# Token tiles of 512 columns in five groups and 448 in the sixth, and a last product by halves of its tokens

## What the kernel computes

```python
qn = q / (norm(q, axis=1) + 1e-06); kn = k / (norm(k, axis=1) + 1e-06)
a  = softmax(kn^T @ qn / tau)            # 256 x 256
x  = (v @ a)                             # 6016 x 256
x  = square(relu(x @ w_in1)) @ w_out1    # d_ff = 2048
y  = leaky_relu(x2 @ w_in2, 0.01) @ w_out2
```

## Time and profile before

| | us |
|---|---|
| median of 3 runs | 1021.57 |
| lowest and highest | 1021.54, 1021.75 |
| the profiled execution | 1021.69 |
| its span, first to last instruction | 1019.9 |
| TensorE busy | 1015.7 |
| VectorE busy | 724.0 |
| ScalarE busy | 673.3 |

### The profile page before, as it was taken

The page is one execution under the profiler, slowest core; times in us unless marked ns, Lnnn a source line. Parts: engine busy times, 40 slices in busy tenths (PEclk is TensorE's granted clock), DMA queues, the critical chain, the costliest instruction groups (busy, mean ns, idle before and its releaser), DMA issues.

```text
span 1019.9 us, 13177 instructions
## 1 busy us (share of the span) xinstructions
PE 1015.7 (100%) x4602; PEld 859.3 (84%) x4602; DVE 724.0 (71%) x1195; ACT 673.3 (66%) x1186; POOL 27.7 (3%) x35
## 2 busy tenths in 40 slices
PE   9999999999999999999999999999999999999998
PEld 8888888888888888888888888888888888888887
DVE  6999766667667666666558777867777777777665
ACT  6898877777777777777665556555555556555454
POOL 3700000000000000000000000000000000000000
PEclk9999999999999999999999999999999999999999
DMA  9800121130130131125361001002002002000001
GB/s 364 315 21 22 32 82 45 54 137 32 67 137 31 68 119 51 68 77 188 116 210 64 1 26 56 1 1 80 1 1 80 1 1 82 1 1 35 6 0 42
DMA packets 33874, 69.27 MB, mean 68 GB/s; under 512 B 2832, under 2 KB 18704, under 8 KB 33808
## 3 DMA queue, kind: packets, MB, share of 16 engines
q1 hardware_dynamic: 33232, 67.25, 18.9%
q10 hardware_dynamic: 576, 1.18, 0.3%
HBM read 44.56 MB, written 23.86 MB: 67 GB/s over the span
## 4 chain that ended last, share of the span: by engine, by line
PE 99%; DMA 0%; ACT 0%; ACTq 0%; issue 0%
PE psum L525 32%; PE psum L526 32%; PE psum L527 32%; PE psum L532 3%; DMA qk<-in_k 0%; ACT out_buf L1004 0%; PE psum L588 0%; PE psum L577 0%; ACTq L728 0%; PE psum L579 0%
## 5 line engine op out<-in xcount | busy, mean ns | idle before, releaser
L867 ACT ACTIVATE g_hi<-g 128x496 fp32r<-128x496 f32 (+1 forms) x384 | 237.3, 618 | 200.8 <-DVE g L1178 76.6
L1168 DVE TENSOR_TENSOR g_lo<-g,g_hi 128x496 fp32r<-128x496 f32 (+1 forms) x384 | 259.9, 677 | 137.5 <-ACT g_hi L867 135.3
L527 PE MATMUL psum<-g_hi,wout_lo 128*128 128x496 f32 (+1 forms) x768 | 295.4, 385 | 0.0
L526 PE MATMUL psum<-g_lo,wout_hi 128*128 128x496 f32 (+1 forms) x768 | 295.4, 385 | 0.0
L525 PE MATMUL psum<-g_hi,wout_hi 128*128 128x496 f32 (+1 forms) x768 | 295.4, 385 | 0.0
L526 PE MATMUL psum<-xop_lo,win_hi 128*128 128x496 f32 (+1 forms) x672 | 258.5, 385 | 0.0
L527 PE MATMUL psum<-xop_hi,win_lo 128*128 128x496 f32 (+1 forms) x672 | 258.5, 385 | 0.0
L525 PE MATMUL psum<-xop_hi,win_hi 128*128 128x496 f32 (+1 forms) x672 | 258.4, 385 | 0.0
L525 PEld LDWEIGHTS psum<-g_hi,wout_hi 128*128 128x128 f32 x768 | 144.2, 188 | 26.6
L527 PEld LDWEIGHTS psum<-g_hi,wout_lo 128*128 128x128 f32 x768 | 144.2, 188 | 26.5
L526 PEld LDWEIGHTS psum<-g_lo,wout_hi 128*128 128x128 f32 x768 | 144.2, 188 | 26.4
(11 more groups left out here) (104 smaller groups left out, 685.8 us busy)
## 6 DMA issues: line engine op xcount, KB each, us to landing
up_parts<-park_up SPq DMA_DIRECT2D x8, 896.0 KB, 4.2
qk<-in_q SPq DMA_DIRECT2D x15, 384.0 KB, 9.7
qk<-in_k SPq DMA_DIRECT2D x13, 384.0 KB, 11.1
stage_o<-in_w_out SPq DMA_DIRECT2D x16, 256.0 KB, 3.4
down_parts<-park_down SPq DMA_DIRECT2D x8, 512.0 KB, 2.8
raw<-in_vT SPq DMA_DIRECT2D x8, 496.0 KB, 4.9
x_tiles<-out_buf SPq DMA_DIRECT2D x8, 496.0 KB, 2.9
raw<-x_tiles SPq DMA_DIRECT2D x8, 496.0 KB, 4.1
```

The lines of the kernel that those rows point to most:

```text
L526: pe.matmul(out, a_hi, b_lo, start=False, stop=False, **more)
L527: last = pe.matmul(out, a_lo, b_hi, start=False, stop=stop and i == len(operands) - 1, **more)
L867: act.activation(g_hi[:, tile, 0:W], g[:, tile, 0:W], ACT.Copy).then_inc(g_hi_made[tile], 1)
L1168: dve.tensor_tensor(g_lo[:, tile, 0:W], g[:, tile, 0:W], g_hi[:, tile, 0:W].bitcast(F32), ALU.subtract).then_inc(g_split[tile], 1)
```

## The change

The widths become five groups of 512 columns and a last one of 448; they add up to the same 3008. Groups 1 to 4 and 7 to 10 get wider, groups 5 and 11 narrower. In the end `down_last` takes the place of `down` for C12: it does o = 0 whole (3 matmuls of 448 columns) and o = 1 in two halves of 224 columns, the second into another PSUM bank (`end_bank`, bank 3), into which ScalarE has first copied what is summed so far. VectorE copies o = 0 of the second tile instead of ScalarE. The halves are copied and stored each by itself, the first by SyncE's queue, the second by ScalarE's.

```diff
-    WIDTHS = [512, 496, 496, 496, 496, 512]
+    WIDTHS = [512, 512, 512, 512, 512, 448]
+    END = width(ALL_GROUPS - 1)
+    def end_tokens(h):
+        return bass.ds(2 * sum(WIDTHS[0:GROUPS - 1]) + END + h * END // 2, END // 2)
+        end_bank = banks[3][:, 0:END // 2]
+        end_seeded = sem("end_seeded")
+        end_done = [sem(f"end_done{h}") for h in range(2)]
 # SyncE, at the end
             for j in range(2):
                 sp.wait_ge(out0_made[j], ALL_GROUPS)
-                sp.dma_start(yT_b[:, 0, tokens(ALL_GROUPS - 1, j)], out_buf[:, 0, j, 0:width(ALL_GROUPS - 1)]
-                             ).then_inc(stored[j], 16)
+                sp.dma_start(yT_b[:, 0, tokens(ALL_GROUPS - 1, j)], out_buf[:, 0, j, 0:END]).then_inc(stored[j], 16)
+                sp.wait_ge(out1_made[j], ALL_GROUPS)
                 if j == 0:
-                    sp.wait_ge(out1_made[j], ALL_GROUPS)
-                    sp.dma_start(yT_b[:, 1, tokens(ALL_GROUPS - 1, j)], out_buf[:, 1, j, 0:width(ALL_GROUPS - 1)]
-                                 ).then_inc(stored[j], 16)
-            for j in range(2):
-                sp.wait_ge(stored[j], 16 * (ALL_GROUPS + 1))
+                    sp.dma_start(yT_b[:, 1, tokens(ALL_GROUPS - 1, j)], out_buf[:, 1, j, 0:END]).then_inc(stored[j], 16)
+                else:
+                    sp.dma_start(yT_b[:, 1, end_tokens(0)], out_buf[:, 1, j, 0:END // 2]).then_inc(stored[j], 16)
+            sp.wait_ge(stored[0], 16 * (ALL_GROUPS + 1))
+            sp.wait_ge(stored[1], 16 * (ALL_GROUPS + 2))
 # TensorE
+            def down_last():
+                m = 2 * (QUADS - 1) + ROW[C12]
+                pe.wait_ge(g_split[C12], WINDOWS)
+                three_passes(acc[0][1][:, 0:END], [(wout_hi[:, m, 0:P], wout_lo[:, m, 0:P], g_hi[:, C12, 0:END],
+                                                    g_lo[:, C12, 0:END])], start=False).then_inc(end_first, 1)
+                pe.wait_ge(end_seeded, 1)
+                for h, place in enumerate((acc[1][1][:, 0:END // 2], end_bank)):
+                    cols = slice(h * END // 2, (h + 1) * END // 2)
+                    three_passes(place, [(wout_hi[:, m, P:C], wout_lo[:, m, P:C], g_hi[:, C12, cols],
+                                          g_lo[:, C12, cols])], start=False, skip_group_check=True
+                                 ).then_inc(end_done[h], 1)
-            for tile in (C11, C22, C21, C12):
+            for tile in (C11, C22, C21):
                 down(WINDOWS - 1, tile)
+            down_last()
 # ScalarE, at the end (out_end and its three calls and the store are taken out)
+            act.wait_ge(down_done[C22], WINDOWS)
+            act.activation(end_bank, acc[1][1][:, END // 2:END], ACT.Copy).then_inc(end_seeded, 1)
+            act.wait_ge(end_first, 1)
+            act.wait_ge(stored[0], 16 * (ALL_GROUPS - 1))
+            act.activation(out_buf[:, 0, 0, 0:END], acc[0][0][:, 0:END], ACT.Copy).then_inc(out0_made[0], 1)
+            act.wait_ge(end_done[0], 1)
+            act.wait_ge(stored[1], 16 * (ALL_GROUPS - 1))
+            act.activation(out_buf[:, 1, 1, 0:END // 2], acc[1][1][:, 0:END // 2], ACT.Copy).then_inc(out1_made[1], 1)
+            act.wait_ge(end_done[1], 1)
+            act.activation(out_buf[:, 1, 1, END // 2:END], end_bank, ACT.Copy).then_inc(out1_made[1], 1)
+            act.wait_ge(out1_made[1], ALL_GROUPS + 1)
+            act.dma_start(yT_b[:, 1, end_tokens(1)], out_buf[:, 1, 1, END // 2:END]).then_inc(stored[1], 16)
 # VectorE, at the end, behind out_second(ALL_GROUPS - 1, 0)
+            dve.wait_ge(end_first, 2)
+            dve.wait_ge(stored[1], 16 * (ALL_GROUPS - 1))
+            dve.tensor_copy(out_buf[:, 0, 1, 0:END], acc[0][1][:, 0:END]).then_inc(out0_made[1], 1)
```

More of the change, by code:

```diff
@@ L638, in down @@
                     cut = slice(o * P, (o + 1) * P)
+                    read_early = Q == WINDOWS - 1 and tile == C22 and o == 1
                     last = three_passes(acc[o][j][:, 0:W], [(wout_hi[:, m, cut], wout_lo[:, m, cut],
@@ L641, in down @@
                                         start=quad == 0 and tile in (C11, C22),
-                                        stop=quad == QUADS - 1 and tile in (C21, C12))
-                    if Q == WINDOWS - 1 and o == 0 and tile in (C21, C12):
+                                        stop=quad == QUADS - 1 and tile in (C21, C12) or read_early)
+                    if Q == WINDOWS - 1 and o == 0 and tile == C21:
                         last.then_inc(end_first, 1)
                 last.then_inc(down_done[tile], 1)
+            def down_last():
[9 more added lines that the diff above has]
+                                 ).then_inc(end_done[h], 1)
             def wait_weights(Q, split):
@@ L995, in _ @@
             g_high(WINDOWS - 1, C12)
[L997 to L1004, removed]
-            out_end(0, 0, out0_made[0])
-            out_end(0, 1, out0_made[1])
-            out_end(1, 1, out1_made[1])
-            act.wait_ge(out1_made[1], ALL_GROUPS)
-            act.dma_start(yT_b[:, 1, tokens(ALL_GROUPS - 1, 1)], out_buf[:, 1, 1, 0:width(ALL_GROUPS - 1)]
-                          ).then_inc(stored[1], 16)
+            act.wait_ge(down_done[C22], WINDOWS)
[10 more added lines that the diff above has]
+            act.dma_start(yT_b[:, 1, end_tokens(1)], out_buf[:, 1, 1, END // 2:END]).then_inc(stored[1], 16)
         @block.vector
```

## The result

The changed kernel takes 1023.65 us (median of 18 runs, 1023.45 to 1024.08) against 1021.67 us for the kernel before (18 runs beside it). The ratio is 1.0018 with a 95% interval of 1.0012 to 1.0025: 2.0 us slower, outside the range that was forecast. The profiled execution has a span of 1021.9 us against 1019.9.

A forecast was written before the change was run, and what follows sets the result against it. TensorE's gapless matmul stream was taken to bound the kernel. Widths 0, group 5 to 6 +0.07, last product +0.04 and tail -0.15 sum to -0.04 us: 1021.65 profiled, 1021.53 median, range 1021.0 to 1022.3 for 8 in 10.

The forecast's parts named there:

- What bounds it, and the count of matmuls and columns: Whole kernel: TensorE's matmuls follow without a gap; 4320 matmuls and 2 x 3008 columns per block stay, 960.0 us before and after.
- The line: TensorE's matmul pitch: columns x 0.4167 ns plus 13.3 ns, drawn through 256, 496 and 512 columns; 200.0 ns at 448, no change.
- the far ends of 0.187 and 0.220: Bounds on the 448-column pitch: no fixed part, 9.6 us less over 720 matmuls; the 496-column pitch, 14.4 us more.
- Rival C: 448-column matmuls wait for their weight load of 188 to 191 ns plus 13.3: 0.203 us each, +2.2 us, 1023.7; chance 0.03.
- The other engines: VectorE and ScalarE chains feeding TensorE at the new widths: distances suffice, nothing lost except +0.07 us where group 5 meets 6.
- group 5 to 6: Windows 48 and 49: distance ahead of S2 falls from 0.43 to 0.18 us; stall 0 to 0.13, taken as +0.07.
- part (c): Windows 48 and 49: narrower downs shorten the time before S2 by 0.32 us, its 512-wide chain only by 0.07; +0.07 us taken.
- Rival B: 448-column windows: VectorE's dependence chain does not shrink with width, 0.21 us missing in each of 16 windows; 3.4 us, 1024.9; chance 0.03.
- The last product: Last product, three matmuls of 448 and six of 224 columns: 1.24 us in place of 1.20, +0.04; at most +0.12.
- The prediction's estimate of 0.120: 224-column matmuls in the last product: weight load of 107 ns plus the fixed part sets the pitch; +0.12 us instead of +0.04.
- The tail: After E, the end of TensorE's stream: last stores at 389 GB/s, span ends E + 3.20 instead of E + 3.42; -0.15 us taken.

## Why the prediction was wrong

- **What bounds it, and the count of matmuls and columns**: right. TensorE's stream is the span, and 512 columns kept 226.67 ns.
- **"The line gives 448 x 0.4167 + 13.3 = 200.0 ns"**: the step that failed. Three widths lie on the line, but they are good widths at the places these tiles have, not samples of a law. At 448 columns the stream takes 202.67 ns, +1.91 us. The sum also put the meeting of two widths at nothing, without a term for it, and it costs another 0.23. I had read the line as interpolation, and gave the far ends of 0.187 and 0.220 no weight in the range; 202.7 lay well within them. The runs show that the excess depends on the width, on what ran before, and on where the tokens lie against the weights.
- **Rival C** had the size (0.203 us a matmul, 1023.7 us) with a chance of 0.03, by another mechanism. Shorter loads leave 448 at 202.2 to 202.3 ns, and 400 columns run at 180.0 under the same loads: it was not the load's length. The row I set against it, a pitch of 0.120 at 256 columns under loads of 191 ns, rightly spoke against a floor, and wrongly closed the question.
- **The other engines**: right. The distances stayed sufficient; of the +0.07 us at group 5 to 6 nothing came, and 0.25 us of distance is enough. The mechanism of part (c) is real all the same: with 400 columns the distance was 0.05 us, and the wait 0.11. Rival B did not happen.
- **The last product**: +0.06 against +0.04, at 0.110 us a matmul. In the streams of 224 columns alone a matmul took 111.5 ns with 128 columns of weights and 103.3 with 64, so there the load counts, and the line's 106.7 is no law at this width either. The prediction's estimate of 0.120, by the length of a load in the Trainium skill, page "TensorE: Matmul & The Clock Gate", section "LDWEIGHTS (loading the stationary operand)", was further off than the line.
- **The tail**: -0.15 forecast, +0.03 found. The issues came at E + 0.58 and E + 0.59, for E + 0.57 and E + 0.68 forecast. Two terms were mis-sized. The rate of 389 GB/s was not kept: from 1019.4 us on the full stretches have 305 to 403, 359 in the mean, and data end at E + 2.37 in place of E + 2.26. The old end has E + 2.37 at this width too, so halves bring no byte in earlier. And 1.09 us follow the last byte in place of 0.94, as in every trace that stores in halves and in none that stores whole. Taken apart, the width gave 0.13 us and the halves took 0.17.
- **The range** was 1021.0 to 1022.3 because the pitch stood in it as known.

What stays open is what happens in TensorE or in SBUF's reading when an excess comes. At 448 columns it is not a delay of a few matmuls among many on the line. The views print starts to 10 ns, but the trace keeps them in whole nanoseconds, and in group 5 of the changed kernel the distances repeat every five matmuls, 199, 207, 202, 203, 202 ns to within 1, 1013 together, which is five times 202.67. The stream of matmuls alone has the same rhythm at 448 columns. Moved by 64 bytes (the narrow groups only) it is 198, 202, 200, three times 200.0. At 488 columns and 225.7 ns the rhythm has seven steps, one of them 241 to 242 ns.

## What to carry to other kernels

- A matmul's time between two measured widths is not known by a line. Time the width itself before a tiling is chosen, in the kernel and behind the widths that will stand before it. A stream of matmuls alone gives a first answer and no more: it had the full kernel's 202.67 ns at 448, but at 488 it had 225.7 where one full kernel had 220.0, at 464 it was 1.1 ns off and at 416 1.6.
- A change of width within the stream has a price of its own, here 0.23 us for four windows, and 0.45 in the kernel with the narrow groups moved.
- A last piece stored in halves by two queues ended 0.17 to 0.25 us later than stored whole.
- Where matmuls bound a kernel and its width changes, look at the mean distance between their starts per group before any wait. An excess of 1% has no gap that a timeline of waits shows.
- Moving a tile by 64 bytes can be worth as much as a change of the tiling, in both directions. It is tried group by group, since a place that is good for 448 columns is bad for 512.

## What the runs showed of the hardware

- float32r matmuls with 128x128 weights took columns x 0.4167 + 13.3 ns to within 0.2 ns at 512, 496 (behind 512), 416 (behind 512), 400, 320 and 256 columns, up to 9.0 ns more at others (488), and 1.7 ns less at 288. bfloat16 took columns x 0.4167 + 2.5 ns at all seven widths tried, 189.2 at 448.
- The excess depends on the place of the tokens in SBUF against that of the weights: 64 bytes changed 202.7 to 200.2 ns at 448 and 226.7 to 230.1 at 512, and 256 bytes changed nothing at 448, 488 and 504. The Trainium skill, page "TensorE: Matmul & The Clock Gate", section "Step-by-step: what each phase is for", says that TensorE has two independent read ports in SBUF and that loading the next weights doesn't steal bandwidth from the running matmul. For float32r the measurements are hard to square with that: a move of the weights alone changed the pitch of the stream from 225.8 to 220.2 ns at 488 columns, and moving both left it as it was (225.3). They show that the two places count together, and not by which path.
- 496 columns has two speeds, 220.0 and 223.3 ns, each kept for 270 matmuls and more. So have 488 (220.0 behind 508, 225.7 behind 496 and 512) and 448 (202.7 behind 512, 206.7 behind 400). Behind 2 matmuls of 448, 496 has 220.0 ns, and behind 4 of them 223.3: which speed comes is decided at the start of the run of that width.
- A store of the last piece in halves by two queues left 1.07 to 1.09 us between the last byte and the end of the span, a store as a whole 0.90 to 0.94.
- The granted clock was 1.00 in all of these stretches, the higher of its two levels.
